# Second inverse DFT of the spectral mixer: rounded passes, a trip through DRAM for the transposes, and a split last DFT

## The reference

```python
X = np.fft.rfft(x, axis=1)                      # x: 2 x 3008 x 256, float32
Xr, Xi = X.real, X.imag
Yr = Xr @ w_r - Xi @ w_i + b_r                  # 256 x 256 weights
Yi = Xr @ w_i + Xi @ w_r + b_i
Yr = np.sign(Yr) * np.maximum(np.abs(Yr) - 0.01, 0.0)
Yi = np.sign(Yi) * np.maximum(np.abs(Yi) - 0.01, 0.0)
y = np.fft.irfft(Yr + 1j * Yi, n=3008, axis=1)
h = y @ w_in;  y2 = (h * np.cos(h)) @ w_out     # 6016 x 256, 256 x 2048, 2048 x 256
h = y2 @ w_in2; out = (h * clip(h + 3, 0, 6) / 6) @ w_out2
```

## Time and profile before

| | us |
|---|---|
| median of 3 runs | 1244.07 |
| lowest and highest | 1243.01, 1246.96 |
| the profiled execution's own time | 1244.57 |
| its span, first to last instruction | 1242.6 |
| PE busy in it | 1224.3 |

### The profile page before, as it was taken

One profiled execution on the slowest core, in us unless ns is written; L12 is line 12 of the kernel. 1 busy time (PEld: TensorE's weight loads), 2 busy tenths in 40 slices (PEclk: granted clock), 3 DMA queues, 4 the chain that ended last, 5 costly groups with the idle time before them and its releaser, 6 DMA issues.

```text
span 1242.6 us, 15601 instructions
## 1 busy us (share of the span) xinstructions
PE 1224.3 (99%) x5872; PEld 1035.4 (83%) x5872; DVE 611.0 (49%) x634; ACT 610.8 (49%) x658; POOL 526.3 (42%) x271
## 2 busy tenths in 40 slices
PE   8999999999999999999999999999999999999998
PEld 8888898778888888888888888888888888888888
DVE  2777745654443544544534444445445445344344
ACT  2566443554444545544554544545455445544443
POOL 2566233444444444444444444444444444444420
PEclk9999999999999999999999999999999999999999
DMA  9022064000010010010100000100100100000000
GB/s 247 27 66 63 15 221 148 3 15 1 1 34 1 1 35 1 0 34 0 34 0 0 34 0 0 34 0 0 34 0 0 34 0 30 0 1 17 1 17 13
DMA packets 23393, 36.01 MB, mean 29 GB/s; under 512 B 2145, under 2 KB 10433, under 8 KB 23362
## 3 DMA queue, kind: packets, MB, share of 16 engines
q1 hardware_dynamic: 23362, 35.58, 9.5%
HBM read 23.25 MB, written 12.32 MB: 29 GB/s over the span
## 4 chain that ended last, share of the span: by engine, by line
PE 94%; DMA 2%; DVE 1%; ACT 1%; POOL 1%; issue 0%; SPq 0%; DVEq 0%
PE banks L508 41%; PE banks L547 40%; PE banks L405 2%; PE banks L406 2%; PE banks L410 2%; PE banks L497 2%; PE banks L452 2%; PE banks L433 1%; PE banks L432 1%; PE banks L389 1%; DMA xb<-in_x 1%; DMA x_spill<-xs 1%; POOL gal L1010 1%; PE banks L487 1%; SPq L273 0%
## 5 line engine op out<-in xcount | busy, mean ns | idle before, releaser
L1010 POOL TENSOR_TENSOR gal<-ga,gah 128x1024 fp32r<-128x1024 f32 (+1 forms) x94 | 225.6, 2400 | 541.0 <-ACT gah L703 541.0
L854 DVE SCALAR_TENSOR_TENSOR phase<-phase,banks 128x1024 f32<-128x1024 int32 (+1 forms) x96 | 114.9, 1197 | 273.9 <-ACT phase L679 273.9
L1016 POOL TENSOR_TENSOR gbl<-gb,gbh 128x1024 fp32r<-128x1024 f32 x88 | 210.5, 2392 | 19.8 <-ACT gbh L737 19.8
L695 ACT ACTIVATE cosine<-phase,half_pi 128x1024 f32<-128x1024 f32 (+1 forms) x96 | 109.1, 1136 | 190.4 <-DVE phase L858 190.4
L679 ACT ACTIVATE phase<-banks 128x1024 int32<-128x1024 f32 (+1 forms) x96 | 97.0, 1011 | 164.8 <-PE banks L508 164.2
L926 DVE SCALAR_TENSOR_TENSOR gb<-ramp,banks 128x1024 f32<-128x1024 f32 (+1 forms) x96 | 115.1, 1199 | 111.8 <-ACT ramp L727 108.1
L887 DVE TENSOR_TENSOR ga<-banks,cosine 128x1024 f32<-128x1024 f32 (+1 forms) x96 | 115.5, 1203 | 110.2 <-ACT cosine L695 95.8
L727 ACT ACTIVATE ramp<-banks,three 128x1024 f32<-128x1024 f32 (+1 forms) x96 | 105.5, 1099 | 116.6 <-PE banks L508 116.6
L737 ACT ACTIVATE gbh<-gb 128x1024 fp32r<-128x1024 f32 (+1 forms) x96 | 100.4, 1045 | 39.1 <-DVE gb L926 34.9
L508 PE MATMUL banks<-xh,w1h 128*128 128x512 f32 (+1 forms) x384 | 117.3, 387 | 0.7 <-issue 0.7
L508 PE MATMUL banks<-xh,w1l 128*128 128x512 f32 (+1 forms) x384 | 117.5, 387 | 0.0
(11 more groups left out here) (92 smaller groups left out, 1824.7 us busy)
## 6 DMA issues: line engine op xcount, KB each, us to landing
xb<-in_x SPq DMA_DIRECT2D x32, 192.0 KB, 6.0
x_spill<-xs SPq DMA_DIRECT2D x16, 376.0 KB, 3.0
xf<-x_spill SPq DMA_DIRECT2D x11, 512.0 KB, 4.4
out_y<-yt SPq DMA_DIRECT2D x11, 512.0 KB, 3.4
wst<-in_w_ff SPq DMA_DIRECT2D x16, 256.0 KB, 2.6
w2st<-in_w_ff SPq DMA_DIRECT2D x16, 256.0 KB, 3.2
dbs<-in_db SPq DMA_DIRECT2D x24, 64.0 KB, 1.7
wmf<-in_w_mix SPq DMA_DIRECT2D x1, 512.0 KB, 7.2
```

The lines of the kernel that those rows point to most:

```text
L695: act.activation(cosine[:, :, 0:w], phase[:, :, 0:w], ACT.Sin, bias=half_pi[:, :], scale=-1.0).then_inc(a_cos, 1)
L854: dve.scalar_tensor_tensor(out=phase[:, :, 0:w], in0=phase[:, :, 0:w].bitcast(i32), scalar=-2.0 * math.pi, in1=bank[:, at:at + 2, 0:w], op ...
L1010: pool.tensor_tensor(gal[p % 2][:, :, 0:w], ga[:, :, 0:w], gah[p % 2][:, :, 0:w].bitcast(fp32), ALU.subtract).then_inc(a_gl, 1)
L1016: pool.tensor_tensor(gbl[pb % 2][:, :, 0:w], gb[:, :, 0:w], gbh[pb % 2][:, :, 0:w].bitcast(fp32), ALU.subtract).then_inc(b_gl, 1)
```

## The change

- `idft2` becomes three rounded matmuls of 512 columns (L493, L494, L496). For that ACT rounds the thresholded values (`ys_high`, L683) and POOL forms the rest (`ys_low`, L1052). The result, `y`, has the 64 real and the 64 imaginary rows of a frequency on partitions.
- `v` and the transposes of stage 3 are gone. Each pass writes its `y` to the DRAM tensor `y_spill` (`write_v`, 128 rows of 2 KB) and reads it back (`read_v`) as two pieces with the frequency on the partition: `v_cos` and `v_sin`. A read of one piece is a DMA into 5 partitions, 12 runs of 2 KB each, and one into 4 partitions, one run each.
- The inverse DFT over 47 is done in 13 groups of 5 (the last of 4) points, each in a sine half and a cosine half of 4 plain float32 matmuls of at most 120 columns. ACT copies both from PSUM (`copy_sine`, `copy_cosine`), DVE forms their sum (`plus`) and POOL their difference (`minus`), which by symmetry are two output points.
- The first layer's weight pieces now go straight to their place, `wf[0]`; POOL forms the low part in place. The second layer's are all loaded in stage 2 and are split on ACT and POOL in steps 0 to 11 of the feed-forward (`w2_hi`, `weights_lo`).
- SyncE's list in stage 2 is now unrolled: for each i, `load_db(i + 2)`, `load_w1(i + 2)`, `write_v(i - 1)`, `read_v(i - 2)`, `load_w2(i - 2)`.

```diff
-SPILL = 2 * BATCH * PN
-SPILLS = TOKENS // SPILL
+HALF = K1
+GROUP = 5
+GROUPS = -(-N2 // GROUP)
+SPILL = BATCH * GROUP * N1
+SINES = 7
+SBUF_S, SBUF_C, SBUF_X = 8, 4, 4
+LAST_K = K1 - 1
...
+    y_spill = nc.dram_tensor("y_spill", [K1, P, BATCH * DIM], fp32, kind="Internal").ap()
...
+        y, y_lo = twice(Region(u_at), "y", [P, K1, BATCH * DIM])
+        r = Region(v_at)
+        v_cos = r.place("v_cos", [P, GROUPS, BATCH * DIM], fp32)
+        v_sin = r.place("v_sin", [P, GROUPS, BATCH * DIM], fp32)
...
+        def w2_chunks(G):
+            if not isinstance(G, int) or G >= PAIRS + NWCH // 4:
+                return ()
+            return (G,) if G < PAIRS else (2 * G - PAIRS, 2 * G - PAIRS + 1)
...
-            def load_db(m, par, reuse):
-                if reuse:
-                    sp.wait_ge(dft2_done, 2 * m + par - 1)
-                sp.dma_start(dbs[par][:, :], db[2 * m + par, :, :]).then_inc(db_in[par], 16)
-
-            def load_weights(j, par, reuse):
-                if reuse:
+            def load_db(i):
+                if i >= 2:
+                    sp.wait_ge(dft2_done, i - 1)
+                sp.dma_start(dbs[i % 2][:, :], db[i, :, :]).then_inc(db_in[i % 2], 16)
+
+            def load_w1(j):
+                if j >= 2:
                     sp.wait_ge(w_hi, j - 1)
-                    sp.wait_ge(w_lo, j - 1)
-                sp.dma_start(wst[par][:, :], w_ff[j, :, :]).then_inc(wst_in[par], 16)
-
-            for par in range(2):
-                load_db(0, par, False)
-            for par in range(2):
-                load_weights(par, par, False)
-            for par in range(2):
-                load_db(1, par, True)
-            with sp.Fori(2, NWCH // 2 + 1) as m:
-                for par in range(2):
-                    load_db(m, par, True)
-                    load_weights(2 * m - 2 + par, par, True)
-            with sp.Fori(NWCH // 2 + 1, K1 // 2) as m:
-                for par in range(2):
-                    load_db(m, par, True)
-
-            sp.wait_ge(w_lo, NWCH)
-            for dst, src in ((c2s, c2), (idn, ident)):
-                sp.dma_start(dst[:, :], src).then_inc(late_consts_in, 16)
+                sp.dma_start(wf[0][:, j * WCH:(j + 1) * WCH], w_ff[j, :, :]).then_inc(w1_in[j % 2], 16)
 
             def load_w2(j):
-                if j >= W2BUF:
-                    sp.wait_ge(w_lo, NWCH + j - W2BUF + 1)
-                sp.dma_start(w2st[j % W2BUF][:, :], w_ff[NWCH + j, :, :]).then_inc(w2st_in[j % W2BUF], 16)
-
-            def spill(tile):
-                sp.wait_ge(xs_ready, 2 * tile + 2)
-                sp.dma_start(x_spill[:, :, tile * SPILL:(tile + 1) * SPILL],
-                             xs[tile % 2][:, :, :]).then_inc(spilled[tile % 2], 16)
+                sp.dma_start(wf[1][:, j * WCH:(j + 1) * WCH], w_ff[NWCH + j, :, :]).then_inc(w2_in, 16)
+
+            def write_v(i):
+                sp.wait_ge(v_ready, i + 1)
+                rows = N2 if i == LAST_K else P
+                sp.dma_start(y_spill[i, 0:rows, :], y[0:rows, i, :]).then_inc(v_out[i % 2], 16)
+
+            def read_v(i):
+                sp.wait_ge(v_out[i % 2], 16 * (i // 2 + 1))
+                full, left = GROUPS - 1, N2 - GROUP * (GROUPS - 1)
+                for dst, rows, at in ((v_sin, K1 - 1, N2), (v_cos, K1, 0)):
+                    if dst is v_sin and i == LAST_K:
+                        continue
+                    done = v_last_in if i == LAST_K else v_in[i % 2]
+                    sp.dma_start(dst[i:i + (GROUP - 1) * rows + 1:rows, 0:full, :],
+                                 y_spill[i, at:at + GROUP * full, :].rearrange("(g r) n -> r g n", r=GROUP)
+                                 ).then_inc(done, 16)
+                    sp.dma_start(dst[i:i + (left - 1) * rows + 1:rows, full, :],
+                                 y_spill[i, at + GROUP * full:at + N2, :]).then_inc(done, 16)
+
+            for i in range(2):
+                load_db(i)
+            for j in range(2):
+                load_w1(j)
+            for i in range(2):
+                sp.dma_start(c2s[i][:, :], c2[i, :, :]).then_inc(c2_in, 16)
+            for i in range(K1 - 2):
+                load_db(i + 2)
+                if i + 2 < NWCH:
+                    load_w1(i + 2)
+                if i >= 1:
+                    write_v(i - 1)
+                if i >= 2:
+                    read_v(i - 2)
+                    if i - 2 < NWCH:
+                        load_w2(i - 2)
+            read_v(K1 - 4)
+            write_v(K1 - 3)
+            write_v(K1 - 2)
+            read_v(K1 - 3)
+            read_v(K1 - 2)
+            write_v(LAST_K)
+            read_v(LAST_K)
...
-                for j in range(BC):
-                    if last and j == DC:
-                        pe.wait_ge(y_ready, K1)
-                    mm = pe.matmul(bank[:, 6 + par, j * P:(j + 1) * P], ys[par][:, j * P:(j + 1) * P],
-                                   ims[:, :], start=True, stop=True)
-                mm.then_inc(idft2_done, 1)
+                o = bank[:, 6 + par, :]
+                pe.matmul(o, imh[:, :], ysh[par][:, :], start=True, stop=False)
+                pe.matmul(o, iml[:, :], ysh[par][:, :], start=False, stop=False)
+                pe.wait_ge(ysl_ready, i + 1)
+                pe.matmul(o, imh[:, :], y_lo[:, bass.ds(i, 1), :].rearrange("p k n -> p (k n)"),
+                          start=False, stop=True).then_inc(idft2_done, 1)
...
-            def turn(q):
-                if q >= 2:
-                    pe.wait_ge(vt_ready, q - 1)
+            m = K1 // 2 - 1
+            mix(m, 0, True)
+            dft2(m - 1, 1, True)
+            idft2(m - 1, 0, True)
+            dft2(m, 0, True)
+            mix(m, 1, True)
+            idft2(m - 1, 1, True)
+            idft2(m, 0, True)
+            dft2(m, 1, True)
+
+
+            def half_idft1(g, at_bank, src, table, rows, done):
+                k, n = part(g) * rows, part(g) * HALF
                 for j in range(BC):
-                    at = (j * N2 + 2 * q)
-                    mm = pe.transpose(bank[0:KC, 4 + q % 2, j * P:(j + 1) * P],
-                                      v[:, at:at + 2, :].rearrange("p n k -> p (n k)"), idn[:, :])
-                mm.then_inc(turned, 1)
-
-
-            def idft1(q):
-                pe.wait_ge(vt_ready, q + 1)
-                if q >= 2:
-                    pe.wait_ge(xs_ready, q - 1)
-                for j in range(BC):
-                    mm = pe.matmul(bank[:, 6 + q % 2, j * P:(j + 1) * P], vt[q % 2][:, j * P:(j + 1) * P],
-                                   c2s[:, :], start=True, stop=True)
-                mm.then_inc(idft1_done, 1)
+                    to = (j % DC * BATCH + j // DC) * n
+                    mm = pe.matmul(bank[:, at_bank, to:to + n], src[0:k, g, j * P:(j + 1) * P],
+                                   table[0:k, 0:n], start=True, stop=True)
+                mm.then_inc(done, 1)
+
+            def sine(g):
+                if g >= 4:
+                    pe.wait_ge(s_copied, g - 3)
+                half_idft1(g, g % 4, v_sin, c2s[1], K1 - 1, sin_done)
+
+            def cosine_part(g):
+                if g >= 4:
+                    pe.wait_ge(plus_done, g - 3)
+                    pe.wait_ge(c_copied, g - 3)
+                half_idft1(g, 4 + g % 4, v_cos, c2s[0], K1, cos_done)
...
-            turn(0)
-            for q in range(1, QN):
-                if q == QN - 1:
+            pe.wait_ge(c2_in, 16 * 2)
+            for par in range(2):
+                pe.wait_ge(v_in[par], 4 * 16 * len(range(par, LAST_K, 2)))
+            sine(0)
+            idft2(K1 // 2 - 1, 1, True)
+            for g in range(1, SINES):
+                sine(g)
+            pe.wait_ge(v_last_in, 2 * 16)
+            for g in range(GROUPS):
+                if g == GROUPS - 2:
+                    pe.wait_ge(s_copied, GROUPS)
                     pe.wait_ge(w_hi, NWCH)
                     pe.wait_ge(w_lo, NWCH)
                     up_a(0, 0)
-                turn(q)
-                idft1(q - 1)
-            idft1(QN - 1)
+                cosine_part(g)
+                if g + SINES < GROUPS:
+                    sine(g + SINES)
...
+            def ys_high(i, par, reuse):
+                act.wait_ge(y_ready, i + 1)
+                if reuse:
+                    act.wait_ge(idft2_done, i - 1)
+                act.activation(ysh[par][:, :], y[:, bass.ds(i, 1), :].rearrange("p k n -> p (k n)"),
+                               ACT.Copy).then_inc(ysh_ready, 1)
...
-            def steps(m, weights, more):
+                if i == 1:
+                    ys_high(0, 0, False)
+
+            def steps(m, weights):
                 for par in range(2):
                     i = 2 * m + par
                     db_high(m, par)
-                    if more:
-                        split_hi(i + 2, par, True)
-                    if more or par == 0:
-                        ab_high(i, par)
-                    else:
```

(58 more changed lines are left out.)

374 lines of the change are left out of this document (191 added, 183 removed).

## The result

| | before | after |
|---|---|---|
| median of the runs, us | 1245.3 (1243.01 to 1246.96, 4 runs) | 1319.34 (1316.97 to 1321.55, 4 runs) |
| ratio | 1 | 1.0596 [1.0565, 1.0626] |
| span of the profiled execution, us | 1242.6 | 1315.2 |

What follows compares the result with a forecast made beforehand. The prediction took PE to bound the kernel, with 94% of the chain. Its terms summed as 1244.57 + 77 - 1.5 - 1 - 12 + 1 + 0.3 = 1308 us, with 1283 to 1332 us holding 8 in 10.

Steps and rivals of the forecast that it cites:

- The loop: Stage 2, ACT's passes 3 to 16: SyncE's order makes each pass wait for the one before; pitch 11.0 us, +77 us.
- ACT's pass, 3.9 us: First part of the loop's pitch in stage 2: ACT's roundings and copies of one pass take 3.9 us.
- Seven issues at 0.43 us, 3.0: Stage 2: SyncE issues seven DMAs before the constants, 0.43 us each, so the constants are issued at 3.2 us.
- Landing at 7.0 us after ACT's end: Stage 2: the constants land at 7.0 us, behind 50 runs on each of five engines taking 4.75 us.
- The waits of ACT: Stage 2: ACT's rounding waits for the constants' DMA 14 times by some 6 to 7 us, 80 to 95 in all.
- The rest of stage two: Stage 2 outside the loop: -1.5 us as PE ends nearer to ACT, -1 us for the seven passes left.
- Stage three, -12: From the end of dft2(22) to the second up: 44.7 us instead of 57.2, -12 us.
- The step itself, 0.89 us: Stage 3: a step of 4 float32 matmuls of at most 120 columns takes 0.89 us.
- The feed-forward, +1: Feed-forward steps: ACT and POOL have room for the second weights; +1 us in case a step's own chain is late.
- The even spread: Rival for stage 2: the reads spread over all engines; pitch 9.5 us, +59 us, 1290 us; chance 0.20.
- Contention: Rival for stage 2: transfers at the slower input-load rate, writes and reads mixing; pitch 12.9 us, +100 us, 1331 us; chance 0.15.
- The rival on the other side: Rival for stage 2: the loop has slack and POOL's order sets the pitch, 5.45 us; 1238 us; chance 0.05.

Runs made afterwards that it cites:

- e1: Changed kernel with weight piece j's DMA waiting for the rounding of piece j-4 instead of j-2 (four semaphores); 1246.22 us, ratio 1.0024.
- e4: Changed kernel with each large read going into 64 partitions, one 2 KB run each, instead of 5 partitions with 12 runs; 1298.12 us, ratio 1.0437.
- e6: e5 with the cosine reads of passes 21 and 22 issued from ACT's DMA queue; 1240.25 us, ratio 0.9974.
- e5: e3 with the first feed-forward step, up_a(0,0), moved behind all cosine steps of stage three; 1240.92 us, ratio 0.9984.
- e7: e6 with the small reads of passes 0 to 10 batched into later turns, two issues fewer per turn with weights; 1242.24 us, ratio 0.9992.
- e10: e8 and e7's edits in one kernel, including e6's second queue; 1237.67 us, ratio 0.9948.
- e8: e5 with the weights' low part in stage two formed on DVE, ahead of ab_lo, instead of on POOL; 1239.28 us, ratio 0.9973.
- e3: e1 with POOL forming y_lo ahead of the weights' low part in each pass; 1243.65 us, ratio 1.0006.
- e9: e8 with DVE's low part of the weights behind ab_lo instead of before it; 1244.5 us, ratio 1.0015.

## Why the prediction was right

**The loop: right, by its named cause.** It forecast +77 us and a pitch of 11.0; measured are +75.7 and 10.98. The wait, its place (L330 on L689), its count of 14, the low clock and the end of it with the weights all came as described. e1 shows that this one wait is 5.7% of the time: its ratio is 1.0024 against 1.0596. Within it, though, three sizes were off and cancelled, so that 10.98 came out so near to 11.0 is luck:

- *ACT's pass, 3.9 us.* It took 3.3. The mean durations of the earlier trace rows are each 0.1 us longer than what an instruction adds behind another.
- *Seven issues at 0.43 us, 3.0.* They took 4.2. The earlier trace rows is a plain load; a read with 5 * 12 runs took 0.74, one of four partitions 0.60.
- *Landing at 7.0 us after ACT's end, for 50 runs on each of five engines.* In the turn shown, a long one, they landed at 92.62, 7.95 after the end of the rounding at 84.67; in the mean turn it is 10.98 - 3.3 = 7.7. The forecast put the transfer as the bound. Measured are 4.2 us of issues and then 3.4 until the landing, of which 1.7 is what a load of the constants took before, so the queue in front adds only about 1.7. Of the 1.5 us that the forecast set between five engines and an even spread, e4 finds 0.5 in the landing and 0.9 in the issues, which the forecast had taken as equal.

The waits of ACT were to be 80 to 95 us in all in 14 times; the twelve of the steady loop were 7.3 to 8.9 us, the fourteen of the loop made 99.3, and all 20 made 106.1. ACT's shorter pass and the longer round trip are the two sides of that.

**The rest of stage two:** -3.2 for -2.5, right in the sum; the runs don't split it into its two terms. PE's own pitch is 4.80.

**Stage three, -12: this term was wrong**, it was -3.2. Three steps of it failed. The first sine step came 17.3 us after `dft2(22)`, not 15: the write took 3.87 us to land behind the reads of passes 19 and 20, SyncE's eight reads of 0.6 to 0.75 us stood behind its landing, and the transfers moved no faster than the issues (e6). With the other shape of the reads it came at 12.2 (e4), so the shape is worth 5 us here, more than in any turn of the loop. The cosines began at 27.8, not 23, by the same trip once more, and since the first sine step ran for 2.04 us at the clock of 0.50 in place of 0.89. And the new order puts a stall that the prediction didn't have in front of the first `up`: `xl` came 4.61 us late, and e5 got 2.7 us back by order alone. The step itself, 0.89 us, was as forecast.

**The feed-forward, +1:** +3.2; which wait took the other 2 us no run tells.

**The total.** 1308 forecast, 1319.34 measured. Of the 11 us, stage three makes 9 and the feed-forward 2; stage two came out 2 lower than forecast; and 2 are between the profiled execution (span 1315.2, own time 1316.97) and the median.

**The rivals.** The even spread (1290) has its own experiment: e4, pitch 9.63 for 9.5, 1298. Of the 9 to 10 us between 1290 and its profiled execution (1299.33), about 4 are stage two, 4 stage three, which took 48.1 us for 43.7, and 2 the feed-forward. Contention (pitch 12.9) did not show: 10.98. The rival on the other side, that the loop has slack and POOL's order is left, is e1: pitch 5.30 for 5.45, 1246 for 1238; its stage three took 55.8 us where 44.7 was forecast. So each case was priced to within 0.2 us of a pitch, and the gain of stage three was forecast too large in all three: by 9 us in the kernel after, 4 in e4 and 11 in e1. The lower clock after a gap, which the forecast used, has its row in the trace before and not in the earlier trace rows: 0.50 from 203 to 205 us.

## What to carry to other kernels

Before pricing a new wait in a DMA-issuing queue, look at what stands behind it in that queue and who waits for it; if the answer leads back to the instruction waited for, the whole round trip enters the pitch, and the durations of the parts matter less than that it closes. Here four semaphores in place of two undid 5.7% of the time, with no work taken away. Then expect the next bound close by: after the first, each single repair gave less than 0.3%. Fewer issues gave nothing while POOL was full (e7); with POOL relieved, e10 came out 0.25% under e8, though it has e6's second queue as well.

## What the runs showed of the hardware

- **The time of an issue depends on the shape.** On SyncE 0.33 to 0.45 us for loads and the write in the turn above, 0.60 for a read into four partitions that lie apart, 0.74 for one of 5 * 12 runs; in e4 0.49 for one into four neighbouring partitions and 0.45 for one into 64. On ACT the first read of e6 took 1.58, the next like it 0.77.
- **A read of 120 KB into 5 partitions is slow in two ways.** It keeps the share of the 16 DMA engines at 0.27 in the mean, where 128 KB into 64 partitions (e4) have 0.50; that is in keeping with five engines and doesn't prove them. What is issued behind it lands later: the constants of a turn after 3.4 us in place of 2.9, the write at the end of stage two after 3.87 in place of 2.02. And it costs issue time, which made 0.9 of e4's 1.35 us a turn.
- **Subtractions of VectorE and GpSimd lengthen each other.** In e3 `ul` on POOL took 2.28 us where it began 0.10 us after DVE's `ab_lo` (77.04 and 76.94), and 1.30 where it began first, 0.11 us ahead of `ab_lo` (71.85 and 71.96); then `ab_lo` took 2.28 in place of 1.22. In e8 POOL's `y_lo` took 2.18 where it began 0.19 us after `ab_lo` (83.86 and 83.67); in e9 DVE's `w_lo` took 1.78 where it began 0.08 us after `y_lo` (79.81 and 79.73). The one that began second grew each time. The Trainium skill, "VectorE: DVE Perf Modes", section "Two Vector instructions with no wait between them", mentions a second SBUF read interface that VectorE shares with GpSimd; that this is the cause no run here shows.
- **The clock.** In the loop, with PE busy for 12.3 to 13.8 of 20 us (80 to 180 us), the granted clock was 0.74 to 0.83 in the mean, and 0.50, the 1.2 GHz level, in the idle stretch of stage three (windows from 235 to 240 us). It was 1.00 throughout 200 to 220 us, when PE had no gaps.
